# Attention, router and experts on one core: zero fill by GpSimd, a shorter index chain, and four batches written out

## The chip, the cores and the metric

The kernel runs on one core of a Trainium2 chip. The metric is the device time of one execution in microseconds. The core has five engines with a queue of instructions each: TensorE (PE, matmuls and transposes), VectorE (DVE), ScalarE (ACT), GpSimd (POOL) and SyncE (SP). Each runs its queue in order; between engines, order is made by semaphores. Data moves between memory (DRAM) and on-chip SBUF by DMA, issued from the queues of SP, POOL and ACT, and carried by 16 DMA engines. Matmul results land in PSUM, eight banks of 512 float32 for each of 128 partitions.

## The reference

```
scores = scale * q @ k.T;  heads 0-3: local mask, heads 4-7: strided mask   # q,k,v [4, 8, 576, 64]
x = softmax(scores) @ v                                        # as rows [2304, 512]
do = x @ w_skip > 0;  e = argmax(x[do] @ w_gate);  gate = softmax(...)[e]   # 8 experts
x[do] += gate * (relu(x[do] @ w1[e]) @ w2[e])                   # w1 [8,512,1024]
g = leaky_relu(x @ w_in, 0.01);  out = g @ w_out                # w_in [512, 2048]
```

## The kernel before

**Attention.** One batch element is 11 groups of work (`GROUPS`): six local ones (96 queries, g = 0 to 5) and five strided ones (126 rows, the last 72, g = 6 to 10), each for four heads. A group goes PE `scores` (L1322 to L1336) -> DVE `scores_less_max` (L1007, L1014) -> ACT `exps` (L804) -> PE `probs` (a transpose, L1348) -> ACT `probs_out` (L813) -> PE `values` (L1361) -> DVE `normalised` (L1023, L1027, L1034, which writes `xo`). The steps of three neighbouring groups are interleaved. Before a group's scores, q and k of its heads must stand transposed in `qt` and `kt`. That is done in 16 chunks for each batch (`CH`): PE transposes a chunk (L1314), ACT or, for those in `ON_DVE`, DVE copies it out of PSUM (L797, L1000); a chunk of k takes two copies, one of q a single one. `CH_AT` says before which group's scores a chunk is done: chunks 0 to 7 of the next batch at groups 7 to 10, chunks 8 to 11 in `head(b)`, the bridge between two batches, and 12 to 15 at groups 2 to 5. The program has the first batch's head, then a loop of three rounds `rest(b); head(b)`, then the last `rest`.

**Loads and stores of the attention.** SP issues them all, in the order of `batch(b, ...)`, L449: after `xo` of group g is written, the store of `xo` to `x_rows` (at g = 2 and 5 one store for three local groups, at each strided group one), the load of v of the next batch for g (one DMA for a local group, four for a strided one, L401), and at g = 2, 4, 6, 8 the loads of q or k of the batch after next (`q_st`, `k_st`). SP runs a loop for the first two batches, and written-out code for the last two. POOL (and ACT, for half of q) copies `q_st` and `k_st` to `q_in` and `k_in`. `xo` has six slots, so DVE's L1034 waits until the store of the group that used the slot before has landed (L1030 to L1033): group 6 waits for the store of groups 0 to 2 of its own batch, group 9 for that of 3 to 5.

**Router and index chain.** `x_rows` is read back (`x_sb`, L441 to L446), transposed, split in two and multiplied with the gate weights for 18 tiles of 128 rows. Then DVE works out, in steps that each wait for the one before (`step`), which expert takes each row, the rank of the row there, and its place in a list of 160-row tiles, eight tiles with fixed places and up to 14 for overflow. Two one-hot tensors (`oh_tok`, `oh_row`) and 18 matmuls (L1470) turn the places into `tok_idx`, the list of rows by half tile. POOL gathers the rows of tile 0 with it (`gather_x`, `s_plan` at 1).

**Experts and MLP.** Each 160-row tile takes 64 matmuls (L1497, L1513) with weights that SP loads a tile ahead, while POOL gathers the next tile's rows, writes the records of `sort_rows`, and loads and splits the weights of the MLP (`stage_load`, `stage_split`). The MLP runs on all 18 tiles of rows with every product in three parts. `y_rows` from row 1120 on must be zero where no expert writes: SP issues one fill of 4800 KB (L481) behind the loads of the last expert weights.

## Time and profile before

| | |
|---|---|
| median of 3 runs | 772.04 us (771.41 to 774.05) |
| profiled execution | 777.4 us, of which the span of the core is 775.2 us |
| attention, first scores to last `xo` | 22.66 to 156.5 us |
| router | 156.5 to 178.9 us |
| index chain and first gather | 178.9 to 202.0 us |
| experts | 202 to 361 us |
| MLP | 361 to 775.2 us |

All times are from the start of the span. A row of a timeline gives start, duration, engine, line, operation, what it writes and reads, how often, and in brackets the idle time ahead with what ended it. SPq is SP's queue: its durations are those of issuing a DMA, not of the transfer.

### The profile page before, as it was taken

The page shows a single profiled execution, that of the slowest core. Times are in us where ns is not written, and L with a number is a line of the kernel's source. Part 1 is how long each engine was busy: PE and PEld are TensorE (multiplying, and loading weights), DVE is VectorE, ACT ScalarE, POOL GpSimd, SP SyncE. Part 2 cuts the span into 40 slices and gives each one's busy share as a digit, 9 for nine tenths or more (in the row PEclk, how much of TensorE's full clock was granted, in tenths as well). Part 3 has the DMA queues.
Part 4 walks back from the last instruction along what each step waited for, and adds up shares of the span by engine and source line. Part 5 has one row for each costly group of instructions (what it writes and reads, how often), then busy time and mean ns, then how long its engine had stood idle before and what let it go on. Part 6 is the DMA issues. An engine that isn't in the chain of part 4 may idle for free.

```text
span 775.2 us, 12846 instructions
## 1 busy us (share of the span) xinstructions
PE 716.9 (92%) x4628; PEld 664.1 (86%) x4628; DVE 276.2 (36%) x578; ACT 262.0 (34%) x522; POOL 180.5 (23%) x182
## 2 busy tenths in 40 slices
PE   2989979993699999998999999999999999999997
PEld 2878868873699999997999999998989899999986
DVE  4667656757100000003332333233333333332222
ACT  4687666651111112212222223322232322222222
POOL 2120100011686666562100310040031004001000
PEclk9999998986699999999999999999999999999999
DMA  8483746779799999972100210030012004001001
GB/s 175 107 188 100 168 102 171 218 236 229 168 317 341 300 314 338 315 248 64 43 1 0 70 54 1 7 116 1 1 59 63 0 0 122 0 0 41 1 0 41
DMA packets 73112, 91.46 MB, mean 118 GB/s; under 512 B 26704, under 2 KB 47728, under 8 KB 73073
## 3 DMA queue, kind: packets, MB, share of 16 engines
q1 hardware_dynamic: 63969, 66.14, 29.7%
q0 software_dynamic: 8048, 24.79, 11.3%
q8 instruction: 24, 0.39, 0.2%
q10 hardware_dynamic: 1056, 0.02, 0.1%
q14 instruction: 15, 0.12, 0.0%
HBM read 73.91 MB, written 17.01 MB: 117 GB/s over the span
## 4 chain that ended last, share of the span: by engine, by line
PE 74%; SPq 10%; DMA 5%; DVE 3%; issue 3%; ACT 2%; another core or an unknown queue 2%; ACTq 0%; DVEq 0%; POOLq 0%
PE psum L1584 26%; PE psum L1603 26%; PE psum L1497 8%; PE psum L1513 8%; SPq L401 6%; DMA x_rows<-xo 3%; SPq L396 2%; SPq L386 1%; ACT kt L797 1%; PE psum L1336 1%; PE psum L1523 1%; PE psum L1566 1%; DMA x_sb<-x_rows 1%; SPq L409 1%
## 5 line engine op out<-in xcount | busy, mean ns | idle before, releaser
L1584 PE MATMUL psum<-x2h,wih 128*128 128x384 f32 x384 | 130.6, 340 | 1.9 <-DVE x2l L1256 1.9
L1274 DVE SCALAR_TENSOR_TENSOR g_act<-g_raw 128x384 f32<-128x384 f32 x96 | 53.6, 558 | 219.4 <-ACT g_raw L960 205.9
L1584 PE MATMUL psum<-x2h,wil 128*128 128x384 f32 x384 | 129.5, 337 | 0.0
L1584 PE MATMUL psum<-x2l,wih 128*128 128x384 f32 x384 | 129.0, 336 | 0.0
L960 ACT ACTIVATE g_raw<-psum 128x384 f32<-128x384 f32 x96 | 47.2, 492 | 235.3 <-PE psum L1584 232.0
L1603 PE MATMUL psum<-woh,g_l 128*128 128x512 f32 x288 | 114.0, 396 | 0.0
L1603 PE MATMUL psum<-wol,g_h 128*128 128x512 f32 x288 | 113.7, 395 | 0.0
L1603 PE MATMUL psum<-woh,g_h 128*128 128x512 f32 x288 | 112.1, 389 | 0.7 <-DVE g_l L1278 0.7
L1497 PE MATMUL psum<-xt,wring 128*128 128x160 f32 x512 | 80.9, 305 | 0.6 <-issue 0.6
L759 POOL DMA_INDIRECT out_dram<-o_sb,idxo x15 | 15.9, 1061 | 277.8 <-ACT o_sb L955 274.8
L1513 PE MATMUL psum<-hp,wring 128*128 128x160 f32 x512 | 77.6, 299 | 0.0
L1584 PEld LDWEIGHTS psum<-x2h,wih 128*128 128x128 f32 x384 | 72.2, 188 | 5.7 <-DVE x2l L1256 2.1
L1584 PEld LDWEIGHTS psum<-x2l,wih 128*128 128x128 f32 x384 | 72.1, 188 | 3.5
L1497 PEld LDWEIGHTS psum<-xt,wring 128*128 128x128 f32 x512 | 74.0, 194 | 0.8 <-ACT xt L886 0.8
L1278 DVE TENSOR_TENSOR g_l<-g_act,g_h 128x384 fp32r<-128x384 f32 x96 | 53.6, 558 | 56.9 <-ACT g_h L965 55.7
L1513 PEld LDWEIGHTS psum<-hp,wring 128*128 128x128 f32 x512 | 72.2, 190 | 0.2 <-ACT hp L906 0.2
L1584 PEld LDWEIGHTS psum<-x2h,wil 128*128 128x128 f32 x384 | 72.0, 188 | 0.0
L965 ACT ACTIVATE g_h<-g_act 128x384 fp32r<-128x384 f32 x96 | 50.3, 524 | 60.1 <-DVE g_act L1274 57.6
L1603 PEld LDWEIGHTS psum<-woh,g_l 128*128 128x128 f32 x288 | 54.0, 187 | 11.5
L1603 PEld LDWEIGHTS psum<-woh,g_h 128*128 128x128 f32 x288 | 54.1, 188 | 10.0 <-issue 0.7
L1603 PEld LDWEIGHTS psum<-wol,g_h 128*128 128x128 f32 x288 | 54.0, 187 | 9.1
L906 ACT ACTIVATE hp<-psum 128x160 f32<-128x160 f32 x64 | 19.2, 304 | 100.5 <-PE psum L1497 97.1
(177 smaller groups left out, 899.2 us busy)
## 6 DMA issues: line engine op xcount, KB each, us to landing
wring<-in_moe_w_dram SPq DMA_DIRECT2D x64, 512.0 KB, 8.6
y_rows<-zrow SPq DMA_DIRECT2D x1, 4800.0 KB
q_st<-in_q_dram SPq DMA_DIRECT2D x8, 576.0 KB
k_st<-in_k_dram SPq DMA_DIRECT2D x8, 576.0 KB
x_sb<-x_rows SPq DMA_DIRECT2D x4, 1024.0 KB, 6.4
stage<-in_moe_w_in_dram POOLq DMA_DIRECT2D x4, 1024.0 KB, 9.0
stage<-in_moe_w_out_dram POOLq DMA_DIRECT2D x4, 1024.0 KB, 9.2
vs<-in_v_dram SPq DMA_DIRECT2D x20, 128.0 KB, 7.6
```

Source lines behind the costliest of these rows:

```text
L396: eng.dma_start(vs[lo:P, g, :, 0:DH], src).then_inc(s_v[g], 16)
L401: eng.dma_start(vs[0:G["m"], g, h, 0:DH], src).then_inc(s_v[g], 16)
L759: pool.indirect_dma_start(out=out, out_offset=bass.IndirectOffsetOnAxis(ap=idxo[:, j:j + 1].bitcast(U32), axis=0), in_=o_sb[:, j, :], in_o ...
L906: act.activation(hp[:, f % 4, :], bank[f % 2][:, 0:TILE], ACT.Relu).then_inc(s_hp, 1)
L960: act.activation(g_raw[:, f % 2, :], bank[f % 2][:, 0:MT * P], ACT.Copy).then_inc(s_mr, 1)
L965: act.activation(g_h[:, f % 2, :], g_act[:, f % 2, :], ACT.Copy).then_inc(s_mh, 1)
L1274: dve.scalar_tensor_tensor(out=g_act[:, f % 2, :], in0=g_raw[:, f % 2, :], scalar=LEAK, in1=g_raw[:, f % 2, :], op0=ALU.mult, op1=ALU.max) ...
L1278: dve.tensor_tensor(g_l[:, f % 2, :], g_act[:, f % 2, :], g_h[:, f % 2, :].bitcast(F32), ALU.subtract).then_inc(s_ml, 1)
L1497: last = pe.matmul(bank[f % 2][:, 0:TILE], wring[:, 2 * u_, w_], xt[:, T.par, c, :], start=(c == 0), stop=(c == KD - 1))
L1513: last = pe.matmul(Y[:, c, 0:TILE], wring[:, 2 * u_ + 1, w_], hp[:, f % 4, :], start=(f == 0), stop=(f == FC - 1))
L1584: last = pe.matmul(bank[f % 2][:, 0:MT * P], wt[:, c, f * P:(f + 1) * P], xp[:, T.par, c, :], start=(c == 0 and n == 0), stop=(c == KD - 1 ...
L1603: last = pe.matmul(bank[4 + j][:, :], gt[:, f % 2, j * P:(j + 1) * P], wt[:, f // 4, w_], start=(f == 0 and n == 0), stop=(f == FC2 - 1 an ...
```

## The change

Three things at once. (1) The fill of `y_rows` is cut in three (`zero_rows`, 1600 KB each) and issued by POOL, each behind POOL's copy of a batch's first half of q. (2) In the index chain the list for the eight fixed tiles is made by a shorter chain of its own (`rank`, `hid0`, `row0`, `eq_b`, `tok_b`, `row_b`); the overflow part (`row_o`, `tok_o`), the records and the sort positions come behind the plan, and 18 matmuls for it stand in PE's first expert tile. POOL's part of the one-hot tensors goes to DVE. The two halves of the logits are added by a matmul with `comb`. (3) The attention is written out for all four batches, on SP too, in one even pipeline: no `head`; chunks 8 to 15 stand at groups 1 to 4; POOL does all copies of q and k but the first ones; at the start q and k of the first half come in two pairs of heads, DVE takes every second chunk, and POOL does one memset of `kt`. SP loads q and k of a batch together, at groups 1 and 6.

```diff
-        CH_AT = {2: [12], 3: [13], 4: [14], 5: [15], 7: [0, 1], 8: [2, 3], 9: [4, 5], 10: [6, 7]}
-        ON_DVE = {9, 11}
+        CH_AT = {1: [8, 9], 2: [10, 11], 3: [12, 13], 4: [14, 15]}
+        CH_NEXT = {7: [0, 1], 8: [2, 3], 9: [4, 5], 10: [6, 7]}
+        def on_dve(b, n):
+            return n % 2 == 1 if b == 0 and n < 8 else n in (9, 13)
...
+            qk_load(sp, 0, 0, q, q_st, s_qs[0], PAIRS[0])
+            qk_load(sp, 0, 0, k, k_st, s_ks[0], PAIRS[0])
+            qk_load(sp, 0, 0, q, q_st, s_q2, PAIRS[1])
+            qk_load(sp, 0, 0, k, k_st, s_k2, PAIRS[1])
...
-                    if qk_ahead and g in (2, 6):
-                        sp.wait_ge(s_qi[g // 6], b + 2)
-                        qk_load(sp, b + 2, g // 6, q, q_st, s_qs)
-                    if qk_ahead and g in (4, 8):
-                        sp.wait_ge(s_ki[g // 8], b + 2)
-                        qk_load(sp, b + 2, g // 8, k, k_st, s_ks)
+                    if b + 2 < B and g in (1, 6):
+                        qk_next(b + 2, g // 6)
...
-            sp.dma_start(y_d[(E - 1) * TILE:SKIP, :].rearrange("(p c) n -> p c n", p=FILL),
-                         zrow[:, :].unsqueeze(1).to_broadcast([FILL, ZC, D])).then_inc(s_zd, 16)
...
+                        pool.tensor_copy(to, what).then_inc(s_in, 1)
+                        if b and hs == 0 and dst is q_in:
+                            zero_rows(b - 1)
...
+                if i == 0:
+                    pool.wait_ge(s_tok_o, 1)
                 stage_split(i)
...
+            step(dve.tensor_tensor(posn[:, :, :], RANK[:, 0:NT, :], ohb[:, 0:NT, 1:E + 1], ALU.mult))
+            step(dve.reduce_sum(rank[:, :], posn[:, :, :], AX.X))
+            dve.scalar_tensor_tensor(out=h80[:, :], in0=rank[:, :], scalar=float(HALF), in1=half2[:, :],
+                                     op0=ALU.is_ge, op1=ALU.add).then_inc(s_r, 1)
...
+            dve.tensor_tensor(eq_b[:, :, :], free(hid0[:, :], HB3, 2), free(c_half[:, 0:HB], HB3, 1),
+                              ALU.is_equal).then_inc(s_eqb, 1)
+            dve.tensor_tensor(row_b[:, 0:NR, :], free(row0[:, 0:NR], R3, 2), free(c_row[:, :], R3, 1),
+                              ALU.is_equal).then_inc(s_rowb, 1)
...
+                    if first and f == 5:
+                        for hf in range(2):
+                            pe.wait_ge(s_xf[hf], 2)
+                        pe.wait_ge(s_hot_o, 3)
+                        for t in range(NT):
+                            last = pe.matmul(TIDX_O, row_o[:, t, :],
```

On SP, at the start of the loop over batches. Before, in the loop (96x3x256 is the store of three local groups, 128x4x64 the v load of a local group, 72x4x512 four heads of q or k):

```order
L396 DMA vs<-in_v_dram 96x4x64
L396 DMA vs<-in_v_dram 128x4x64
L386 DMA x_rows<-xo 96x3x256
L396 DMA vs<-in_v_dram 128x4x64
L409 DMA q_st<-in_q_dram 72x4x512
L396 DMA vs<-in_v_dram 128x4x64
```

The change, at the same place (SP's rows 17 to 23):

```order
L427 DMA vs<-in_v_dram 96x4x64
L427 DMA vs<-in_v_dram 128x4x64
L440 DMA q_st<-in_q_dram 72x4x512
L440 DMA k_st<-in_k_dram 72x4x512
L417 DMA x_rows<-xo 96x3x256
L427 DMA vs<-in_v_dram 128x4x64 x3
L417 DMA x_rows<-xo 96x3x256
```

The loads of q and k, one behind the first store and one behind the load at g = 4 before, now both stand ahead of that store.

On PE in the first expert tile of the change (L1501 is the hidden layer, L1517 the output share, L1484 the turn of the next tile's rows, L1553 the new matmuls):

```order
L1484 MATMUL psum<-ident,xg 128x80 x8
L1501 MATMUL psum<-xt,wring 128x160 x4
L1517 MATMUL psum<-hp,wring 128x160 x4
L1501 MATMUL psum<-xt,wring 128x160 x4
L1517 MATMUL psum<-hp,wring 128x160 x4
L1553 MATMUL psum<-tok_o,row_o 80x56 x18
L1501 MATMUL psum<-xt,wring 128x160 x4
```

The overflow list is now made inside the tile, behind its sixth hidden step; before, all matmuls of the list stood ahead of the tile (L1470, 80x88 x18).

## Rows read from the trace of the kernel before

**Rows 1.** The page: TensorE's granted clock in 40 slices of 19.4 us
```profile
PEclk9999998986699999999999999999999999999999
```

**Rows 2.** Stretches: busy of each engine, granted clock, DMA share and rate
```profile
22.66:156.50 133.84, 117.84 (x1134) 111.84 (x1132) 90.39 (x231) 93.49 (x165) 17.02 (x9) 0.95 0.60 152
178.90:202.00 23.10, 4.94 (x47) 4.13 (x46) 15.78 (x55) 2.01 (x4) 6.04 (x6) 0.57 0.88 211
```

**Rows 3.** Timeline of SP's queue, the first store and the q load behind it
```profile
37.26 0.37 SPq L386 DMA_DIRECT2D x_rows<-xo  x1
...
38.46 2.92 SPq L409 DMA_DIRECT2D q_st<-in_q_dram  x1
```

**Rows 4.** DMA issues of the stretch 37.2:37.3, KB and us to landing
```profile
x_rows<-xo SPq DMA_DIRECT2D x1, 288.0 KB, 8.3
```

**Rows 5.** The stretch 34.6 to 54.6 (columns as in rows 2)
```profile
34.60:54.60 20.00, 16.37 (x165) 15.28 (x164) 11.55 (x31) 17.23 (x30) 4.30 (x3) 1.00 0.85 194
```

**Rows 6.** Timeline of DVE: xo of (batch, group) (0, 6), (2, 3), (3, 0), (3, 10)
```profile
49.85 0.42 DVE L1034 TENSOR_TENSOR xo<-psum,den 126x256 f32<-126x256 f32 x1
...
110.55 0.42 DVE L1034 TENSOR_TENSOR xo<-psum,den 96x256 f32<-96x256 f32 x1 [5.18 <-DMA x_rows<-xo]
...
135.99 0.42 DVE L1034 TENSOR_TENSOR xo<-psum,den 96x256 f32<-96x256 f32 x1
...
156.08 0.42 DVE L1034 TENSOR_TENSOR xo<-psum,den 72x256 f32<-72x256 f32 x1
```

**Rows 7.** Timeline of SP's queue, four v loads in the loop, and written out
```profile
105.43 3.71 SPq L401 DMA_DIRECT2D vs<-in_v_dram  x4
...
131.81 3.14 SPq L401 DMA_DIRECT2D vs<-in_v_dram  x4
```

**Rows 8.** Groups of instructions on ACT, 31.5 to 64.5 (one batch)
```profile
L797 ACT ACTIVATE kt<-psum 64x288 f32<-64x288 f32 x14 | 9.4, 670 | 0.3 <-PE psum L1314 0.2
L804 ACT ACTIVATE sc<-sc 96x512 f32<-96x512 f32 (+2 forms) x12 | 7.3, 610 | 5.6 <-DVE sc L1014 5.5
L813 ACT ACTIVATE pt<-psum 128x384 f32<-128x384 f32 (+2 forms) x11 | 5.9, 535 | 0.8 <-PE psum L1348 0.7
...
L842 ACT ACTIVATE q_in<-q_st 72x1024 f32<-72x1024 f32 x2 | 2.1, 1050 | 0.8 <-DMA q_st<-in_q_dram 0.8
```

**Rows 9.** Timeline of the start: two copies on DVE, the third group's scores
```profile
6.33 1.44 DVE L989 COPY q_in<-q_st 72x2048 f32<-72x2048 f32 x1 [2.55 <-DMA q_st<-in_q_dram]
...
13.42 1.16 DVE L989 COPY q_in<-q_st 72x2048 f32<-72x2048 f32 x1
...
26.50 0.42 PE L1327 MATMUL psum<-maskb,identb 96*96 96x512 bf16 x1
```

**Rows 10.** Timeline of the index chain on DVE, PE and POOL
```profile
179.06 0.33 DVE L1097 COPY ls<-psum 128x162 f32<-128x162 f32 x1 [1.83 <-PE psum L1441]
...
183.99 0.28 DVE L1126 TENSOR_TENSOR ovc<-psum,c_over 128x112 f32<-128x112 f32 x1 [0.52 <-PE psum L1460]
...
186.21 0.31 DVE L1141 TENSOR_TENSOR posn<-posn,ohb 128x144 f32<-128x144 f32 x1
...
187.11 0.18 DVE L1146 TENSOR_SCALAR hq<-slot 128x18 f32<-128x18 f32 x1
...
188.44 0.90 DVE L1159 TENSOR_TENSOR oh_row<-row,c_row 128x720 bf16<-128x720 f32 x1
...
192.16 0.85 PE L1470 MATMUL psum<-oh_tok,oh_row 128*80 128x88 bf16 x9 [1.10 <-DVE rec L1163]
...
194.62 1.20 POOL L667 DMA_INDIRECT xg<-x_rows,tok_idx  x1 [2.61 <-issue]
```

**Rows 11.** Timeline of the first expert tile, PE and POOL
```profile
199.99 1.42 PE L1480 MATMUL psum<-ident,xg 80*128 80x80 f32 x8 [6.98 <-DMA xg<-x_rows,tok_idx]
...
202.03 5.38 PE L1497 MATMUL psum<-xt,wring 128*128 128x160 f32 x24 [0.63 <-issue]
...
211.56 4.53 POOL L612 TENSOR_TENSOR wil<-stage,wih 128x2048 fp32r<-128x2048 f32 x1
```

More of the change, by code:

```diff
@@ L436, in x_load @@
+            qk_load(sp, 0, 1, k, k_st, s_ks[1])
+            for g in range(3, NL):
+                v_load(sp, 0, g)
+            qk_next(1, 0)
+            for g in range(NL, NG):
+                v_load(sp, 0, g)
+            qk_next(1, 1)
             def x_load(b):
@@ L447, in x_load @@
                                  ).then_inc(s_x[b], 16)
-            def batch(b, qk_ahead, v_ahead):
+            for b in range(B):
                 for g in range(NG):
@@ L828, in rest @@
-            def rest(b, last):
-                for s_ in range(2, NG):
-                    for n in CH_AT.get(s_, []):
-                        if n >= 8:
-                            chunk(b, n)
-                        elif not last:
-                            chunk(b + 1, n)
-                    probs_out(b, s_ - 2)
-                    exps(b, s_)
-                    if s_ in (6, 8) and not last:
-                        act.wait_ge(s_tq, len(CH) * b + len(CH))
-                        act.wait_ge(s_qs[1], 16 * b + 32)
-                        to, what = heads_in(q_in, q_st, 1)
-                        h2 = slice(s_ // 8 * 2, s_ // 8 * 2 + 2)
-                        part = act.activation(to[:, :, h2, :], what[:, :, h2, :], ACT.Copy)
-                        if s_ == 8:
-                            part.then_inc(s_qi[1], 1)
@@ L850, in _ @@
                 chunk(0, n)
-            act.wait_ge(s_vz, 4)
-            head(0)
-            with act.Fori(0, B - 1) as b:
-                rest(b, False)
-                head(b)
-            rest(B - 1, True)
+            for b in range(B):
+                for g in range(NG):
+                    for n in CH_AT.get(g, []):
+                        if b == 0 and n == 8:
+                            act.wait_ge(s_kz, 1)
+                        chunk(b, n)
+                    for n in CH_NEXT.get(g, []):
+                        if b + 1 < B:
+                            chunk(b + 1, n)
+                    if NG * b + g >= 2:
+                        probs_out(*divmod(NG * b + g - 2, NG))
+                    exps(b, g)
+                    if b == 0 and g == 1:
+                        act.wait_ge(s_wg, 32)
+                        act.activation(wgs[:, :, 0:E + 1], wg[:, :, :], ACT.Copy).then_inc(s_wgh, 1)
             for g in (NG - 2, NG - 1):
@@ L1409, in _ @@
             pe.wait_ge(s_cst, POOL_MASKS)
-            head(0)
-            with pe.Fori(0, B - 1) as b:
-                rest(b, False)
-                head(b)
-            rest(B - 1, True)
+            for b in range(B):
+                for g in range(NG):
+                    for n in CH_AT.get(g, []):
+                        chunk(b, n)
+                    for n in CH_NEXT.get(g, []):
+                        if b + 1 < B:
+                            chunk(b + 1, n)
+                    if g in (0, NL):
+                        copied(b, 15 if g else 7)
+                    scores(b, g)
+                    if NG * b + g >= 2:
+                        probs(*divmod(NG * b + g - 2, NG))
+                    if NG * b + g >= 3:
+                        values(*divmod(NG * b + g - 3, NG))
             probs(B - 1, NG - 2)
```

551 lines of the change are left out of this document (273 added, 278 removed).

## The prediction

> **What bounds the kernel now.** I read the stretches of the stages first. The change touches what lies ahead of 202 us; behind it, experts and MLP follow one another on PE, and what comes earlier there moves everything behind it by as much. In the attention [rows 2] PE is busy 118 of 134 us and ACT 93, with a granted clock of 0.95, so nothing is at its limit on average. The waits say what is: DVE's write of xo for batch 2, group 3 sat 5.18 us until a store had landed [rows 6], and the clock's slices show 0.8 and 0.6 there [rows 1]. The store was late because SP was: in the loop four v loads take SP 3.71 us against 3.14 where the code is written out [rows 7], and a strided group has a store of about 0.9 besides, against 2.0 us for a group on the engines: the last batch, with few chunks left, goes from its first xo at 135.99 to its last at 156.08 [rows 6], ten groups in 20.1 us. Of the engines ACT is the fullest per batch: 14 copies of k at 0.67, 7 of q at about the same, 12 exps at 0.61, 11 copies at 0.535 and 2.1 us of q_in [rows 8], 29 us of the 33 looked at. In the index chain [rows 2] PE has 4.9 of 23 us: DVE's one-by-one steps are the path up to the first gather at 194.62, then the gather itself up to 199.99, then tile 0 at 202.03 [rows 10, 11].
>
> **The start.** The first q copy begins when 576 KB have landed, at 6.33, and PE reaches the third group's scores at 26.50 [rows 9]. With pairs of heads the first data are there after 288 KB, and every second chunk is copied by DVE beside ACT. Worked out in turn (load, copy, two transposes, copy, ...), the first scores come at some 15 us; but the third group now has chunks 10 and 11 ahead of it, whose k lands near 18 behind the same bytes as before and is copied by POOL (1.9 us by its present copies): some 20.8. So the pipeline is 5.7 us earlier.
>
> DVE's copies now run beside POOL's memset of kt. The row beside POOL's memsets is 1.44 us, the one without 1.16 [rows 9]: 0.3 us a copy. The Trainium skill (SBUF — State Buffer, "Who interferes with whom") says that such a copy and a GpSimd instruction shut each other out for the whole instruction; by that a copy could wait out the whole memset, about 2 us as DVE does it now. The row shows 0.3, and I take 0.3, which is inside the rounding of the 5.7.
>
> **Most of it is given back at the first store.** xo of group 6 waits for the store of groups 0 to 2. That store was issued at 37.26 and landed 8.3 us later, at 45.5 [rows 3, 4], 4.3 us ahead of xo (0, 6) at 49.85 [rows 6]. SP gets there no earlier now: its 20 strided v loads of batch 0 are issued ahead of it as before. And both loads of q and k for batch 2 now stand ahead of the store, which stood behind it. They are 1.18 MB, at 194 GB/s in this stretch [rows 5] 6 us: the store lands at 51.4. Without it xo (0, 6) would come at 42 (5.7 earlier, and 2 from ACT's lighter load). So DVE, and two groups later PE, stand for some 9 us, and at this point the change is 1.6 us behind.
>
> **From there to the end of the attention.** ACT per batch: 16 copies of k (10.7), 6 of q (4.0), 11 exps (6.7), 11 copies (5.9): 27.3 us against 29. By slots: groups 1 and 2 together 1 q, 4 k and two groups' 2.3 = 5.7, groups 3 and 4 the same, 7 and 8 with 2 q 6.3, 9 and 10 6.0, and 0, 5, 6 three times 2.05 = 6.2: 29.9, and I add 0.4 for the coupling: 30.3 us a batch. From xo (0, 6) to (3, 6) three of these, 90.9, less 2 for what PE and ACT had done ahead in the stall, less 3.2 for the chunks that the last batch has none of, and 7.0 for the four groups left: 92.7, so 144.1. SP needs some 26 us a batch written out and catches up. Further waits for stores I put at 4.5: about 1 at the second batch's group 1 (its slot's store is behind q and k again), 2.5 at its group 6, 1 at the end as now. The attention ends at 148.6 instead of 156.1: **-7.5**. The router (22.4 us) moves with it.
>
> The loops go away on every engine. PE's rows run over the loop's end without a gap that the views show, so I take nothing. The Trainium skill (Runtime: NRT & Kernel Launch, "Instruction fetch mechanics") says that a taken branch out of the fetched window stalls for a fetch; by that rule three such stalls more would go, without a price there.
>
> **The zero fill.** It runs from 167 to 198, at a DMA share of 0.88 and 211 GB/s [rows 2], so a third, 1.64 MB, is 7.8 us of the engines' time. Nothing waits for it now but the gather beside it (5.4 us from issue to PE's first transpose, [rows 10, 11]); alone I take 0.5 less. Moved into the attention (DMA share 0.60, [rows 2]), the first third falls into the slow strided loads, the second and third beside q and k loads. Nothing if they fit the gaps; at most 7.8 each. I put them within the 4.5 above.
>
> **The index chain.** Before the ranks two steps on the logits and two of the choice go, one small one comes: 4 x 0.34 (0.31 and its wait, [rows 10]) less 0.2 = **-1.2**. Behind the ranks it takes 183.99 to some 193.5 to the list, 9.5. Now: two steps of 144 (0.68), five small ones (0.2 each, overlapped, 0.7), eq_b 0.35, row_b 0.82, tok_b 0.37, row_b 0.82 (half a row of 0.90, its overlap taken off), 9 matmuls 0.85, two small 0.45, handover 0.2: 5.3. **-4.2**. With the gather's 0.5, tile 0 starts **5.9** earlier against the router's end, at 196.1 on the old scale. The steps put behind the plan end at about 200.1 on that scale (some 12 us from 188.1); PE first needs them (s_rec, ahead of the first share) three hidden steps into the tile: 196.1 + 5.4 = 201.5. Hidden, with 1.4 us to spare; without it, that much.
>
> **Tile 0 pays.** 18 more matmuls on PE, at the 0.085 of [rows 10] (0.85 for 9, less its drain) 1.5, and a handover: **+1.7**. POOL's first split waits for the list: it ran 209.55 to 216.1 [rows 11] and would end at some 218.3 on the scale on which PE's need of the next gather is at 226.2; the gather takes 2.4 of issue and 6 to land: 227. **+0.8**.
>
> **The sum.** -7.5 - 5.9 + 1.7 + 0.8 = -10.9 from the profiled execution's 777.4 (span 775.2): 766.5. The runs' median is 772.04; the same difference from it gives **761.1 us**.
>
> **The rivals.** (a) Stores don't bind (chance 0.22): DMA takes the mixed load at more than the 194 GB/s, the store lands by 42. Then no 9 us stall and no 4.5: the attention ends near 138, -18, and the time is 750.5. For it: the chain's stretch, with more than one kind of transfer, has 211 GB/s [rows 2], more than the 194. Against: SP's q load of 38.46 took 2.92 us to issue [rows 3], a full queue. (b) The fill is on the path (0.19): the second and third part each delay the stores by most of their 7.8, 7.5 in all: the attention ends as now, and only the chain's 3.4 is left, 768.6. The Trainium skill (SBUF — State Buffer, "A bandwidth-pool intuition that's wrong (but worth ruling out)") adds that a GpSimd DMA can wait for its descriptors beside VectorE's copies; that would shift a part of the fill later. (c) Slower (0.05): each of the last two parts holds the q and k queue for its whole 7.8, the stores behind fall late in each batch, PE idles, and its clock falls as it did at 113 [rows 1], 3 us each. It decides when waits beyond mine pass 10.9 us: 15.6 of fill and an episode of 3 less the 4.5 give 14.1, 775. (d) Nothing measurable (0.03): the same, stopped between, near 771.
>
> **How the numbers follow.** My own case (0.51) has 756 to 767. The range is to leave out 2 in 10: half of (a) and most of (c) and (d), with (b) inside: 751 to 769. A difference of 0.3%, 2.3 us, is about what a measurement of this kernel can tell. Faster by more 0.93, within 0.03, slower 0.04.
>
> **What would show it.** Scores of the third group near 21; the first store landing near 51 with DVE waiting several us for x_rows<-xo at xo (0, 6); xo (3, 10) near 148; one gap of 5 us or less at (2, 3) gone; POOL's gather 10 us behind the logits; no DMA at 200 GB/s in the chain; 18 matmuls of some 1.5 us in tile 0. The prediction is wrong if the store lands by 45 (then (a)), or if xo waits in each batch for stores behind the fill.

## The result, and the profile after

The changed kernel takes **789.94 us** (median of 4 runs, 788.99 to 791.18) against 771.81 us (4 runs, 771.41 to 774.05) of the kernel before: a ratio of 1.023, with a 95% interval of 1.0203 to 1.0256. It is 2.3% slower, where 761.1 us and 1.4% faster were forecast. The profiled execution took 789.15 us, its span 787.1.

The stretches of the changed kernel first: attention up to the router's first transpose, router up to the logits, chain up to tile 0, tiles up to the MLP. Each row has busy us of the engines, granted clock, DMA share and GB/s.

```profile
16.00:172.50 156.50, 123.92 (x1145) 117.68 (x1143) 86.71 (x229) 93.63 (x165) 28.44 (x17) 0.92 0.65 171
172.50:197.60 25.10, 24.97 (x180) 21.56 (x180) 11.97 (x19) 12.45 (x27) 2.62 (x16) 0.88 0.50 164
197.60:213.25 15.65, 4.87 (x46) 4.08 (x47) 13.21 (x51) 1.73 (x4) 3.12 (x4) 0.55 0.17 48
213.25:372.00 158.75, 155.27 (x1182) 154.21 (x1182) 21.81 (x46) 31.88 (x92) 100.34 (x73) 0.99 0.87 280
```

The attention's last xo comes at 172.06 instead of 156.08 [rows 6]: +16.0 us. The router takes 25.1 instead of 22.5 (156.56 to 179.06), the chain from the logits to tile 0 15.6 instead of 23.0 [rows 2, 10, 11]. From tile 0's first hidden matmul to the end of the span it is 573.8 us, against 573.2. 16.0 + 2.6 - 7.3 + 0.6 is 11.9, the difference of the two spans; the medians differ by 18.1, because the profiled execution of before was a long one of its kind (777.4 against 771.8).

Most of that length lies in the attention. Three later runs (`e4_chain_alone`, `e6_chain_split`, `e10_fill_after_gather`, see below) have the attention of before unchanged, and their last xo comes at 151.90, 151.59 and 151.63, 4.2 to 4.5 us ahead of 156.08. Here the last xo of the change, and that of `e6_chain_split`:

```profile
172.06 0.42 DVE L1049 TENSOR_TENSOR xo<-psum,den 72x256 f32<-72x256 f32 x1
```

```profile
151.59 0.42 DVE L1062 TENSOR_TENSOR xo<-psum,den 72x256 f32<-72x256 f32 x1
```

Against such an execution the attention lost some 20 us and not 16. So the chain did what it promised, and the attention lost more than twice that. The timeline of DVE shows where (xo that waited longest, the time that it waited at the end):

```profile
57.20 0.42 DVE L1049 TENSOR_TENSOR xo<-psum,den 126x256 f32<-126x256 f32 x1 [11.04 <-DMA x_rows<-xo]
...
97.61 0.42 DVE L1049 TENSOR_TENSOR xo<-psum,den 126x256 f32<-126x256 f32 x1 [6.71 <-DMA x_rows<-xo]
...
121.13 0.42 DVE L1049 TENSOR_TENSOR xo<-psum,den 96x256 f32<-96x256 f32 x1 [5.67 <-DMA x_rows<-xo]
```

and the view of waits adds them up, for the changed kernel (16 to 172.5 us), with total, times and longest:

```profile
DVE xo L1049 <- DMA x_rows<-xo: 34.0, 10, 11.0
```

and for the kernel before (16 to 156.5 us):

```profile
DVE xo L1034 <- DMA x_rows<-xo: 8.0, 6, 5.2
```

The xo buffer waits 34 us for its stores, where it waited 8. The stores are late because SP, which issues them, is. Its timeline in the changed kernel:

```profile
17.14 22.64 SPq L432 DMA_DIRECT2D vs<-in_v_dram  x20
...
42.37 0.49 SPq L440 DMA_DIRECT2D q_st<-in_q_dram  x1
42.90 0.54 SPq L440 DMA_DIRECT2D k_st<-in_k_dram  x1
43.48 2.92 SPq L417 DMA_DIRECT2D x_rows<-xo  x1
```

and of the kernel before, the same 20 loads:

```profile
17.15 17.39 SPq L401 DMA_DIRECT2D vs<-in_v_dram  x20
```

Two things are to be read there. The 20 strided loads of v took 22.64 us; those of the kernel before, begun at the same time, took 17.39, and its first store went out at 37.26 [rows 3]. And both loads for batch 2 stand ahead of the store, as the prediction said. The store landed at 57.1, not 51.4. While SP worked through the 20 loads, the first third of the fill was in flight. Pool issued it at 24.5, and from issue to landing the three thirds took, by the view of its tile:

```profile
DMA to landing us min/median/max: 12.3/13.7/16.5
```

where the sum had counted 7.8 us each.

### The profile page after: what moved, and what is told of

It reads as the page before. It is cut to its first block, busy times and chain, and to the rows that moved or that the text cites. A ratio compares the mean times of both kernels' runs of the same rounds, so it can differ in the third digit from the quotient of the medians.

```text
span 787.1 us, 12509 instructions
## 1 busy us (share of the span) xinstructions
PE 725.5 (92%) x4664; PEld 673.9 (86%) x4664; DVE 273.8 (35%) x590; ACT 256.7 (33%) x515; POOL 194.1 (25%) x192
## 4 chain that ended last, share of the span: by engine, by line
PE 80%; SPq 6%; DMA 5%; DVE 4%; ACT 2%; issue 2%; ACTq 0%; DVEq 0%
PE psum L1599 26%; PE psum L1618 25%; PE psum L1517 9%; PE psum L1501 9%; DMA x_rows<-xo 5%; SPq L432 4%; PE psum L1378 2%; PE psum L1399 2%; ACT kt L846 2%; PE psum L1440 1%; PE psum L1457 1%; PE psum L1350 1%; SPq L440 1%; PE psum L1527 1%; PE psum L1581 1%
## 5 line engine op out<-in xcount | busy, mean ns | idle before, releaser
L805 POOL DMA_INDIRECT out_dram<-o_sb,idxo x15 | 15.9, 1062 | 278.8 <-ACT o_sb L982 275.7
L1501 PE MATMUL psum<-xt,wring 128*128 128x160 f32 x512 | 80.5, 304 | 0.7 <-issue 0.6
L1517 PE MATMUL psum<-hp,wring 128*128 128x160 f32 x512 | 77.5, 299 | 0.3 <-DVE pos_i L1224 0.3
L1501 PEld LDWEIGHTS psum<-xt,wring 128*128 128x128 f32 x512 | 73.5, 193 | 1.2 <-issue 1.2
L1517 PEld LDWEIGHTS psum<-hp,wring 128*128 128x128 f32 x512 | 72.1, 190 | 0.5 <-issue 0.5
L1399 PE MATMUL psum<-vs,pt 128*96 128x65 f32 (+2 forms) x352 | 42.1, 267 | 16.8 <-DVE xo L1049 14.7
```

Of the source, the lines that this page charges most:

```text
L805: pool.indirect_dma_start(out=out, out_offset=bass.IndirectOffsetOnAxis(ap=idxo[:, j:j + 1].bitcast(U32), axis=0), in_=o_sb[:, j, :], in_o ...
L1399: last = pe.matmul(OP[n % 2][0:G["m"], h, :], pt[0:G["w"], n % 2, h, 0:G["m"]], vs[0:G["w"], g, h, :], start=True, stop=True)
L1501: last = pe.matmul(bank[f % 2][:, 0:TILE], wring[:, 2 * u_, w_], xt[:, T.par, c, :], start=(c == 0), stop=(c == KD - 1))
L1517: last = pe.matmul(Y[:, c, 0:TILE], wring[:, 2 * u_ + 1, w_], hp[:, f % 4, :], start=(f == 0), stop=(f == FC - 1))
```

## The experiments

Three theories. **F**: the fill in the attention slows SP's queue, and with it loads and stores. **O**: the order of the loads does it, q and k ahead of the store. **P**: the pipeline written out evenly is itself slower than the loop. All ratios are to the kernel before, run beside each on the same chip; its median there was 771.8 us beside the change and 772.3 to 773.7 beside the others. Times within a stage come from one profiled execution of each kernel, and three of them (`e1_fill_back`, `e2_order_back`, `e15_back_spread`) have their first xo 1.5 us or more later than the other profiles of the new attention, for a reason told under "The start" below; so differences of a stage of some 2 us between runs mean little.

One thing changed beside what the runs are named for. The fill of before and of `e4_chain_alone`, `e6_chain_split`, `e10_fill_after_gather` and `e11_fill_last` writes 20 rows from each of 120 partitions (`ZC = 20`); to be divisible by three it is 24 rows from each of 100 in the change and in all the others. Both move some 180 to 230 GB/s, but the DMA share from 180 to 184 us is 0.92 in before and 0.63 in `e3_both_back`.

### Fill and order, put back one by one

`e1_fill_back` leaves the changed kernel as it is, but the fill is SP's again, in one piece behind the last weights:

```diff
+            sp.dma_start(y_d[(E - 1) * TILE:SKIP, :].rearrange("(p c) n -> p c n", p=FILL),
+                         zrow[:, :].unsqueeze(1).to_broadcast([FILL, ZC, D])).then_inc(s_zf, 16)
-                        if b and hs == 0 and dst is q_in:
-                            zero_rows(b - 1)
```

> The changed kernel (789.9 us) with the zero fill taken out of the attention: SP issues it in one piece behind the last expert weights, as before. Theory F (the fill keeps the DMA rings full while v, q, k and the stores go by; the first store then lands at 57 instead of 51): the first strided v loads take SP 17.4 us again instead of 22.6, the first store lands near 51.5, the waits of xo for stores fall from 32.6 us in all to about 12, and the time falls by 17 to 21 less 0.5 for the gather beside the fill: 770 to 773. Theory O (the order of q, k and store on SP is the cause, the fill lies in gaps): the waits stay above 25 us and the time at 784 or more.

`e2_order_back` leaves the fill with Pool and puts the loads at their old places:

```diff
-                    if b + 2 < B and g in (1, 6):
-                        qk_next(b + 2, g // 6)
+                    if b + 2 < B and g in (2, 6):
+                        sp.wait_ge(s_qi[g // 6], brought_in(b + 1, g // 6))
+                        qk_load(sp, b + 2, g // 6, q, q_st, s_qs[g // 6])
+                    if b + 2 < B and g in (4, 8):
+                        sp.wait_ge(s_ki[g // 8], brought_in(b + 1, g // 8))
+                        qk_load(sp, b + 2, g // 8, k, k_st, s_ks[g // 8])
```

> The changed kernel with the loads of q and k of the batch after next where they stood before: q behind groups 2 and 6, k behind groups 4 and 8; the fill stays with POOL in the attention. Theory O: the first store lands 6 us earlier (near 51), the wait of 11 us at the first batch's group 6 falls to about 5, those at group 1 of the second and third batch (4.2 and 5.7) go, and so 15 us or more: 772 to 776. Theory F: the stores still stand in full rings behind the fill; 5 us or less are won: 785 or more.

`e3_both_back` has both edits:

> Both of these edits together: attention written out in the even pipeline, short index chain, but fill and order of the loads as before. If fill and order are all that was wrong, the waits for stores fall to about 5 us and the time to 757 to 763, faster than before (771.8). If the even pipeline is itself slower than the old one with its heads (theory P), it stays at 768 or more with few waits of xo.

Measured, with the last xo and the waits of xo for stores from each profile (new order first):

| | median us | ratio (95%) | last xo | waits for stores |
|---|---|---|---|---|
| the change | 789.94 | 1.0230 (1.0203-1.0256) | 172.1 | 34.0 |
| e1: fill back | 779.55 | 1.0077 (1.0050-1.0104) | 156.2 | 11.4 |
| e2: order back | 785.21 | 1.0176 (1.0150-1.0201) | 165.6 | 23.1 |
| e3: both back | 774.73 | 1.0032 (1.0008-1.0056) | 150.3 | 3.8 |

The fill costs 10.4 us with the new order and 10.5 with the old one; the order costs 4.7 with the fill in the attention and 4.8 without it (by the ratios, which take out that the change ran on another chip, 11 to 12 and 3.5 to 4). The two add up, and both F and O are right, F for at least twice as much. The 20 loads of v show F without any store in play. In `e1_fill_back`:

```profile
17.34 17.66 SPq L432 DMA_DIRECT2D vs<-in_v_dram  x20
```

and in `e2_order_back`, where the third is in flight again:

```profile
17.66 21.89 SPq L432 DMA_DIRECT2D vs<-in_v_dram  x20
```

But with both put back the kernel isn't faster than before, though chain and start are in it. So something is left. P has a part of it: the attention ends at 150.3, only 1.3 us ahead of the loop of before. The gather has another: issued at 183.92, it met the fill, and tile 0 started 13.1 us behind it, against 7.4 in the profile of before.

### The chain alone, the fill alone

`e4_chain_alone` is the kernel before with the new index chain and comb (the parts of the change's diff behind the attention), nothing else:

```diff
-                        last = pe.transpose(LOG[:, 2 * j + u, :], lt[:, j % 2, u * P:(u + 1) * P],
-                                            ident[0:LW, 0:LW])
+                        last = pe.matmul(LOG[:, 2 * j + u, :], lt[:, j % 2, u * P:(u + 1) * P],
+                                         comb[:, :], start=True, stop=True)
...
-            step(dve.tensor_copy(ls[:, :, :], LOG[:, :, 0:E + 1]))
-            step(dve.tensor_tensor(ls[:, :, :], LOG[:, :, E + 1:LW], ls[:, :, :], ALU.add))
```

> The kernel before with the index chain of the change alone (comb matmul, short list, overflow list in tile 0); attention and fill as before. The traces put the chain at 15.6 us from logits to tile 0 against 23.0, the router at 25.1 against 22.6 and the MLP the same: 7.3 less 2.5 is 4.8, and the fill beside the gather may give back 0.5: 767.0 to 768.0. If the gather had gained mainly because the fill was gone, 769 or more.

773.44 us (10 runs, 771.62 to 776.21), ratio 1.0008 (0.9992 to 1.0025): no measurable difference. Its gather on Pool, and PE's first transpose of each half and first hidden matmul:

```profile
187.33 1.22 POOL L685 DMA_INDIRECT xg<-x_rows,tok_idx  x1 [31.32 <-issue]
...
194.62 0.79 PE L1525 MATMUL psum<-ident,xg 80*128 80x80 f32 x4 [8.83 <-DMA xg<-x_rows,tok_idx]
...
197.77 0.80 PE L1525 MATMUL psum<-ident,xg 80*128 80x80 f32 x4 [2.35 <-DMA xg<-x_rows,tok_idx]
...
199.14 1.14 PE L1542 MATMUL psum<-xt,wring 128*128 128x160 f32 x3 [0.57 <-issue]
```

The gather goes out 10.0 us behind the logits (177.35), where it was 15.6 [rows 10]. But tile 0 starts 11.8 us behind it, where it was 7.4 [rows 10, 11]. In the changed kernel that is 5.8 (207.49 to 213.25). The gain of the chain (5.6 us) is there, and the gather gives 4.4 of it back, as long as the fill, behind the weights, is still running. The comb matmul, which the edit brings along, costs something too: from the last xo to the logits it is 25.5 us here and 23.0 in before.

`e5_fill_alone` is the kernel before with only the fill moved to Pool's loop:

```diff
-            sp.dma_start(y_d[(E - 1) * TILE:SKIP, :].rearrange("(p c) n -> p c n", p=FILL),
-                         zrow[:, :].unsqueeze(1).to_broadcast([FILL, ZC, D])).then_inc(s_zd, 16)
...
                     pool.tensor_copy(to, what).then_inc(s_in, 1)
+                    if hs == 0 and dst is q_in:
+                        zero_rows(b)
```

> The kernel before with one part alone: the zero fill in three parts from the Pool queue during the attention. Theory D (the transfers of a third slow the SP queue's loads by 4.5 to 5 us in each of three batches, whatever loop order stands around them): the attention ends some 15 us later, the first gather has the DMA engines to itself and gives 2 us back, 784 to 788 us, and the 20 strided v loads of batch 0 take 21 to 23 us instead of 17.4. Rival L (only the new loop is so sensitive; the old one has room between its q and k loads): 772 to 778 us.

790.08 us (4 runs, 788.87 to 792.67), ratio 1.0224 (1.0188 to 1.0261). That is as much as the whole loss of the change and a little more than theory D expected; rival L falls. The loop of before isn't hardier than the new one: its last xo comes at 170.72, some 19 us later than in the three profiles without this fill. Its SP:

```profile
17.14 22.70 SPq L402 DMA_DIRECT2D vs<-in_v_dram  x20
```

`e12_fill_half` asks whether it is the bytes or the issues: half the rows in three parts from Pool, half from SP at the end. Its diff against `e5_fill_alone`:

```diff
-                c0 = b * (ZC // (B - 1))
+                c0 = b * (ZC // (2 * (B - 1)))
+            sp.dma_start(part[:, ZC // 2:ZC, :], zrow[:, :].unsqueeze(1).to_broadcast(
+                [FILL, ZC // 2, D])).then_inc(s_zd, 16)
```

> The kernel before with the fill divided: half of its rows in three parts of half the size from Pool in the attention, the other half from SP behind the weights. The whole of it in the attention gave 790.1 us. Theory D, proportional (bytes cost what they take from the DMA engines): half of 17 to 19 us, 779 to 783 us. Rival T (the loop has slack, and only what goes beyond it costs): under 776 us. Rival Q (each issue costs, by whatever size, the queue of Pool or an interruption): 786 us or more.

779.83 us (4 runs), ratio 1.0103 (1.0071 to 1.0135): +7.5 us for half the bytes, +17 for all. That is proportional within the intervals, as D says; T and Q, as they were put, fall. Some slack isn't excluded: the attention ends at 158.1, 6.5 us later than without a fill in it, for half the bytes, and 19 for all, and the 20 loads took 18.68 us, where they took 16.3 to 17.9 in the runs without and 22.7 with a whole third. The half parts landed after 7.2 to 8.8 us.

### Where else the fill could go

`e6_chain_split` (the chain alone, the fill in two halves on two queues):

```diff
+        def zero_half(eng, u):
+            c0 = u * (ZC // 2)
+            part = y_d[(E - 1) * TILE:SKIP, :].rearrange("(p c) n -> p c n", p=FILL)
+            eng.dma_start(part[:, c0:c0 + ZC // 2, :], zrow[:, :].unsqueeze(1).to_broadcast(
+                [FILL, ZC // 2, D])).then_inc(s_zd, 16)
...
+            zero_half(sp, 0)
...
+            zero_half(act, 1)
             act.wait_ge(s_sh, 1)
```

> The short chain alone in the kernel before, as in the run where it was worth nothing (773.4 us), but the zero fill goes out in two halves, one behind the weights on SP's queue and one on ScalarE's queue after the last router copy. Theory G (the shorter chain is worth nothing because its gather meets the fill, which moves only some 210 GB/s on one queue and ends at 195 to 199 us): the fill is through by about 190 us, the first gather's tile is turned 3.4 to 5 us after its issue instead of 7.3, and the time falls to 767 to 770 us. Rival W (the fill is limited by what it writes, not by its queue): it still ends at 195 us or later, and the time stays at 772 to 774 us.

772.04 us (10 runs), ratio 0.9982 (0.9962 to 1.0002). Mostly rival W: packets of the fill were seen up to some 191 us (193 in `e4_chain_alone`), and the gather issued at 185.11 was turned from 192.48 on, 7.4 us later, as in `e4_chain_alone`. The two queues together moved little more than one does; the first stretch is of `e6_chain_split`:

```profile
176.00:190.00 14.00, 3.28 (x38) 2.93 (x38) 11.68 (x48) 0.67 (x2) 3.04 (x3) 0.54 0.92 230
```

and this one of the kernel before:

```profile
176.00:198.00 22.00, 6.10 (x59) 4.70 (x57) 16.52 (x57) 2.77 (x7) 5.86 (x5) 0.64 0.90 210
```

`e10_fill_after_gather` (loop of before, short chain without comb) holds the fill until the gather has landed:

```diff
+            for hf in range(2):
+                sp.wait_ge(s_gx[hf], 16)
+            sp.dma_start(y_d[(E - 1) * TILE:SKIP, :].rearrange("(p c) n -> p c n", p=FILL),
+                         zrow[:, :].unsqueeze(1).to_broadcast([FILL, ZC, D])).then_inc(s_zd, 16)
             tile(0, 0)
+            sp.wait_ge(s_zd, 32)
```

> The loop of the kernel before, the short chain with the logits turned and added (no comb), and the whole zero fill issued by SP only once both halves of the first gather have landed, waited for after tile 0. Theory G (the chain's gain is taken by the fill that the gather meets): the first gather's tile is turned 3 to 4 us after its issue and the first hidden matmul of tile 0 comes 16 us after the logits instead of 20 to 22. Theory D (the DMA engines were 0.98 busy in the tile stretch, so a fill there delays weights): the stretch of the tiles takes 3 to 12 us longer than 149 us. Together 768 to 778 us; under 768 would speak against D there, and a first gather that still takes 7 us or more against G.

780.12 us (4 runs), ratio 1.0105 (1.0074 to 1.0137), and it shows both sides. The gather, as G says:

```profile
183.71 1.21 POOL L684 DMA_INDIRECT xg<-x_rows,tok_idx  x1 [27.96 <-issue]
```

```profile
186.91 0.79 PE L1525 MATMUL psum<-ident,xg 80*128 80x80 f32 x4 [4.75 <-DMA xg<-x_rows,tok_idx]
...
189.58 2.74 PE L1542 MATMUL psum<-xt,wring 128*128 128x160 f32 x9 [0.57 <-issue]
```

3.2 us to the first transpose, 5.9 to tile 0. And the tiles, from the first to the last hidden matmul, as D says:

```profile
189.58:351.40 161.82, 154.56 (x1138) 153.65 (x1138) 16.97 (x38) 28.96 (x85) 100.76 (x74) 0.95 0.98 302
```

In the kernel before this stretch is

```profile
202.03:351.73 149.70, 149.00 (x1119) 148.47 (x1120) 12.18 (x22) 28.53 (x85) 99.77 (x73) 0.99 0.94 291
```

12.1 us less. PE was idle for 7.3 us of the longer stretch and for 0.7 of the other, and its matmuls took 5.6 us more, at a granted clock of 0.95 against 0.99. All of it is lost ahead of 230 us: SP's queue stood behind the fill, its next four weight loads took from 194.38 to 215.94 to issue, and from 230 us on PE is busy throughout. So this edit shows the price of a fill ahead of weights on SP's queue; a fill on another queue at this place wasn't tried.

`e11_fill_last` issues it all from Pool in the last batch:

```diff
+            pool.wait_ge(s_xo, NG * (B - 1) + 4)
+            pool.dma_start(y_d[(E - 1) * TILE:SKIP, :].rearrange("(p c) n -> p c n", p=FILL),
+                           zrow[:, :].unsqueeze(1).to_broadcast([FILL, ZC, D])).then_inc(s_zf, 16)
             pool.wait_ge(s_xo, NG * B)
```

> The same kernel with the whole zero fill issued by Pool in the fourth batch, after its fourth group (some 140 us), where the v loads are nearly all issued and no later batch waits for a store. Theory D: the fill is through at 165 to 170 us, beside stores, row loads and weights; the last batch and the router lose 1 to 4 us in all, and the gather gives 4 to 6 us back: 767 to 772 us. Rival (the fill does as much harm there as in the first three batches, by the stores of the last groups and the row loads of the router): 776 us or more.

789.74 us (4 runs), ratio 1.0222 (1.0187 to 1.0257). My expectation failed, and the rival is right: the fill took 32.0 us to land, and one xo waited 20 us for a store beside it:

```profile
172.77 0.42 DVE L1057 TENSOR_TENSOR xo<-psum,den 126x256 f32<-126x256 f32 x1 [20.08 <-DMA x_rows<-xo]
```

That the last batch has few loads to issue doesn't help: its xo buffer has as few places as in the others, and a store that lands late stops it.

### The pipeline itself

`e8_pipe_split` is the changed kernel with the old order of loads (as in e2), the fill in two halves at the end (as in e6), and the logits turned and added as before (the diff of e4 the other way round).

> The changed kernel with the q and k loads at their old places, the zero fill in two halves (SP's and ScalarE's queue) at the end of the attention, and the logits turned and added as before instead of multiplied by comb. From the run of both put back (774.7 us): if theory G holds 5 to 6 us less from the gather, and 1 us less from the router (1.8 us of comb's matmuls less 0.7 us of two adds on VectorE), so 767 to 769 us; without G 773 to 774 us. The router then takes 23.7 us from the last xo to the logits, as before, plus nothing.

773.62 us (10 runs), ratio 1.0019 (0.9999 to 1.0039). Stores hardly bind here (1.3 us in all), so this profile shows the pipeline bare, and from one batch's first xo to the next it takes 33.3 us, not the 30.3 of the prediction:

```profile
61.60 0.42 DVE L1057 TENSOR_TENSOR xo<-psum,den 96x256 f32<-96x256 f32 x1
...
94.91 0.42 DVE L1057 TENSOR_TENSOR xo<-psum,den 96x256 f32<-96x256 f32 x1
```

The loop of before takes 31.8 where no store holds it (`e6_chain_split`, second batch, first xo at 65.68 and 97.49). Why is seen on ACT and PE in slot 8, where both chunks of a k pair stand:

```profile
79.25 2.77 ACT L852 ACTIVATE kt<-psum 64x288 f32<-64x288 f32 x4
```

```profile
82.08 0.42 PE L1379 MATMUL psum<-maskb,identb 96*96 96x512 bf16 x1 [1.78 <-ACT kt L852]
```

Four copies in a row, and PE waits for ACT until they are done. In the changed kernel each of slots 2, 4, 8 and 10 has such a pair; the loop of before has them in slots 8 and 10 and once at the batch's start, between other work.

`e9_pipe_slots` puts chunks 8 to 11 into the first slot and 12 to 15 one to a slot, as before (and gives DVE chunks 9 and 11 instead of 9 and 13):

```diff
-        CH_AT = {1: [8, 9], 2: [10, 11], 3: [12, 13], 4: [14, 15]}
+        CH_FIRST = {1: [8, 9], 2: [10, 11], 3: [12, 13], 4: [14, 15]}
+        CH_LATER = {0: [8, 9, 10, 11], 2: [12], 3: [13], 4: [14], 5: [15]}
```

> The same as the pipeline with the two halves of the fill, with one change: from batch 1 on the chunks 8 to 11 of q and k stand in the first slot of the batch and 12 to 15 one to a slot in slots 2 to 5, as in the kernel before, instead of two to a slot in slots 1 to 4. Theory S (two chunks in each of slots 1 to 4 make these slots longer, 33.3 us a batch against 31.9 in the old loop): 1.4 us less in each of three batches, 3 to 5 us less than the other pipeline run. Rival E (the batch is set by the DMA side, loads and stores, wherever the chunks stand): within 1 us of it.

774.41 us (10 runs), ratio 1.0012 (0.9994 to 1.0029), and 34.1 us a batch (97.29 to 131.43): theory S in this form is wrong. Four chunks in one slot of an even pipeline are no better than two in four; the loop of before had probs and values between them.

`e13_pipe_spread` changes only the tables against `e8_pipe_split`, so that no slot has a whole k pair:

```diff
-        CH_AT = {1: [8, 9], 2: [10, 11], 3: [12, 13], 4: [14, 15]}
-        CH_NEXT = {7: [0, 1], 8: [2, 3], 9: [4, 5], 10: [6, 7]}
+        CH_FIRST = {1: [8, 9], 2: [10, 11], 3: [12, 13], 4: [14, 15]}
+        CH_LATER = {0: [8], 1: [9, 10], 2: [11], 3: [12, 13], 4: [14], 5: [15]}
+        CH_NEXT = {6: [0], 7: [1, 2], 8: [3, 4], 9: [5, 6], 10: [7]}
```

> The pipeline run with the fill in two halves at the end (773.6 us, 33.3 us from batch to batch without a wait for a store), with the chunks spread so that no slot has both halves of a k pair: 8, 9+10, 11, 12+13, 14, 15 in slots 0 to 5 from batch 1 on, and 0, 1+2, 3+4, 5+6, 7 in slots 6 to 10. Theory K (two k chunks in one slot are four copies, 2.8 us in a row on ScalarE, and TensorE waits 0.9 to 1.8 us for them three times a batch): 31.5 to 32 us a batch, 768 to 770 us. Rival (the wait only moves to other slots): 33 us a batch and 773 us.

**763.70 us** (4 runs, 761.8 to 768.41), ratio 0.9879 (0.9843 to 0.9915). The one batch without a wait for a store takes 29.8 us (31.5 and 33.2 the other two):

```profile
92.98 0.42 DVE L1061 TENSOR_TENSOR xo<-psum,den 96x256 f32<-96x256 f32 x1
...
122.83 0.42 DVE L1061 TENSOR_TENSOR xo<-psum,den 96x256 f32<-96x256 f32 x1
```

and PE's waits for ACT's copies of q and k fell from 14.0 us in `e8_pipe_split` to 8.8 in the attention. The placement is worth more than I expected of it: 1.4 points of ratio against `e8_pipe_split`, 10 us, and 7.7 us when the kernel ran again (below). PE's shorter waits for copies of k are what theory K said. But the tables also spread the chunks over all 11 slots instead of 8, and no run parts the two. Waits for stores rose in turn from 1.3 to 9.7 us; the next limit is there.

(CH_FIRST is for batch 0, CH_LATER for the others.) The last three runs take this apart: `e14_after_spread` is the change with these tables, `e15_back_spread` is `e3_both_back` with them, `e16_spread_again` is `e13_pipe_spread` once more.

> The changed kernel with one thing different: the chunks of q and k spread over the slots (8, 9+10, 11, 12+13, 14, 15 in slots 0 to 5 from batch 1 on; 0, 1+2, 3+4, 5+6, 7 in slots 6 to 10). Theory K adds to the fill's cost (each of three later batches is 1.5 to 3 us shorter, whatever the DMA side does): 780 to 785 us. Theory D alone (with the fill and the new load order the batch is set by the DMA engines, and a faster loop only waits longer for its stores): 787 us or more.

788.95 us (4 runs), ratio 1.0196 (1.0148 to 1.0243), no measurable difference from the change. K adds nothing there, and D alone is right: the stores are waited for 31.7 us instead of 34.0. A faster loop only waits longer.

> The changed kernel with fill and load order put back and the chunks spread; the fill in one piece, the logits by comb. Without the spread this was 774.7 us. If the placement carries the gain of the spread run: 764 to 767 us. If the two halves of the fill and the plain logits carry a part of it: 768 to 772 us.

769.09 us (7 runs), ratio 0.9929 (0.9901 to 0.9957), against 1.0032 of `e3_both_back`: the placement carries 1 point (5.6 us by the medians, 8 by the ratios).

> The spread run again, for its size: with the fill in two halves and no comb, 763 to 766 us, 1 to 2 us less than the run without these two, since its router is 1.2 to 1.6 us shorter and two adds on VectorE of 0.35 us each come back.

765.91 us (6 runs, 764.01 to 767.14), ratio 0.9888 (0.9854 to 0.9922). The kernel of `e13_pipe_spread` again: **1.1% faster than the kernel before**, and 3.2 us less than `e15_back_spread` on the same chip, more than I put on comb and the halves. Which of the two has the rest wasn't tried; the router's part, by the profiles, is 23.8 us from the first transpose to the reduce with comb (`e15_back_spread`) and 22.1 without. `e15_back_spread` is one of the profiles that started late; whether its other executions did, no row shows.

## Why the prediction was wrong

**The failed step** is "Further waits for stores I put at 4.5", with the fill's price inside it ("Nothing if they fit the gaps; at most 7.8 each. I put them within the 4.5 above"). The waits after the first were 23 us (34.0 less 11.04), and the fill in the attention costs 15 to 19 us of attention, as the ends of e1 against the change (15.9), e3 against e2 (15.3) and e5 against the three profiles with the attention of before (some 19) show. The bound of 7.8 each was taken from a stretch in which the fill ran with little beside it; beside SP's loads a third landed after 12.3 to 16.5 us. A DMA share of 0.6 looked like room for it. It wasn't: in `e12_fill_half` already half the bytes cost 7.5 us. The prediction's own sign of being wrong, "if xo waits in each batch for stores behind the fill", came. Rivals (b) and (c) named the mechanism: (b), given 0.19, had 7.5 us for it and 768.6 in all; (c), given 0.05, took the fill at 15.6, near what was measured, but set it off against 4.5 of other waits, kept all other gains and came to 775 us. (c) reads its fall of the clock "at 113" from rows 1, and the prediction reads "0.8 and 0.6 there"; in slices of 19.4 us the 0.8 is 116 to 136 us, but the two of 0.6 are 174 to 213, router and chain, and say nothing of a wait for a store. (Shorter stretches do show 0.50 from 114 to 120 us.)

**The base.** The 7.5 us that the attention was to gain were taken off a profile whose attention ended 4.5 us late. A part of that were waits that the same code has less of in other executions: xo (2, 3) waited 5.18 us there [rows 6], 3.39, 1.34 and 1.39 in `e4_chain_alone`, `e6_chain_split` and `e10_fill_after_gather`. So what "one gap of 5 us or less at (2, 3) gone" could give was in part not there to be had, and setting the same difference against the median hid it.

**"SP gets there no earlier now"**, so the store lands at 51.4: right that q and k ahead of it cost 6 us (xo (0, 6) comes at 57.20 with the new order and at 51.21 with the old one in `e2_order_back`; without the fill at 52.62 and 46.81), wrong that SP was as fast as before. It came 6.2 us later (43.48), 5.3 of them in the 20 loads, and the store landed at 57.1. The wait was 11.0 us for 9, and it began at 46.2 and not at 42: where no store holds it, in `e8_pipe_split`, xo (0, 6) comes at 45.50.

**"30.3 us a batch"**: 33.3 for the placement of the change. The sum had ACT's work right (27.3 us a batch) but took ACT as busy throughout the slots that have chunks; the k pairs make PE wait, and ACT then waits for PE. With the chunks spread 29.8 was measured in one batch. In `e3_both_back` the two errors met: no first stall of 9 us, but 3 us more a batch, and it ended at 150.3, near the forecast 148.6. This agreement is chance.

**The order of the loads** I priced once, at the first store. It costs 4.7 us in all, also in later batches (xo (1, 6) waits 6.71).

**The start** was right: third scores at 20.53, forecast some 20.8. But the 0.3 us that a copy beside POOL was to cost was luck. In the changed kernel DVE's four copies from `q_st` and `k_st` took 0.69, 0.69, 0.69 and 0.77 us, because none of them met the memset of `kt` (6.99 to 9.11). In the profile of `e1_fill_back`, where the program's start is the same, the second one did, and took 2.65 us:

```profile
6.53 2.12 POOL L633 MEMSET kt<- 128x2432 f32 x1
```

```profile
6.55 2.65 DVE L1067 COPY k_in<-k_st 72x1024 f32<-72x1024 f32 x1 [1.15 <-DMA k_st<-in_k_dram]
```

It was the same in `e2_order_back` (2.57) and `e15_back_spread` (2.41), whose first xo also come late (30.57 and 30.65, and 30.64 in `e1_fill_back`, against 28.3 to 29.0 in the others). Where the copy came first, the memset was the longer one: 2.55 us in `e3_both_back` and 2.65 in `e9_pipe_slots`. The Trainium skill (SBUF — State Buffer, "Who interferes with whom") states that such a copy can take the ports that VectorE shares with GpSimd, and that whichever issues first has them for the whole instruction while the other is fully blocked. These rows agree. The row of 1.44 us in before agrees too, against how the prediction read it: that copy began at 6.33 inside a memset of POOL that ended at 6.69, and the next, of 80x46 elements, begun at 6.75, took 1.09 us, where it takes 0.13 in the changed kernel. The 0.3 was what was left of a short memset.

**The chain** was right in itself (5.4 forecast; 5.6 from the logits to the gather's issue), but "the gather's 0.5" was mis-sized, and it decides what the chain is worth. With the fill out of the way the gather and its turning take 5.8 us to tile 0, beside it 7.4 in before, 11.8 in `e4_chain_alone` and 13.1 in `e3_both_back`. In `e3_both_back`, `e4_chain_alone` and before, packets of the fill are seen up to 197, 193 and 198 us, though the gather goes out at 183.9, 187.3 and 194.6; a gather issued earlier meets more of it. (Whether the fill from 100 partitions holds a gather longer than that from 120 wasn't tried by itself: to PE's first transpose the gather took 8.0 to 11.2 us beside the first and 5.4 to 7.4 beside the second.) In the changed kernel chain and gather together gave 7.3, forecast 5.9.

**The router** "moves with it (22.4)": missed. comb's matmuls are four instructions of 0.61 us for a pair of tiles

```profile
180.93 0.61 PE L1447 MATMUL psum<-comb,lt 18*128 18x9 f32 x4
```

where before there were two of 0.29 together:

```profile
164.41 0.29 PE L1441 MATMUL psum<-ident,lt 18*128 18x18 f32 x2
```

Over nine pairs that is 2.9 us more of PE, near the 2.6 measured; the two steps that it saves on DVE are 0.7.

**Tile 0 pays**: 0.84 us for the 18 matmuls against 1.7, and no stall at the second gather against 0.8. The step behind the plan was late by 0.31 us. All small.

## What to carry to other kernels

A mean DMA share of 0.6 isn't room for a background transfer where one queue issues loads and stores in order: price the transfer by its bytes (17 us for 4.9 MB here), and read from the issue times of that queue (17.4 against 22.7 us for the same 20 loads) what stands behind it. A transfer that hides behind a serial chain sets a floor for what a shorter chain is worth, if the chain ends in a DMA of its own. And in a pipeline of slots spread the jobs so that no slot gives one engine a long run of them (here four copies, 2.8 us); moving chunks between slots was worth 1% here, once the DMA side left room for it. Before a forecast is taken off one profile, compare it with the median of its kernel: here 5 us of the profile were that execution's own.

## What the runs showed of the hardware

- With the fill in flight the core moved 210 GB/s on one queue and 230 on two (rows above), and two ended it only some 2 us sooner, while 397 GB/s were moved in the stretch 168 to 171 us of `e1_fill_back`, where weights were still coming. In the last batch, beside stores and row loads, the fill's 4.9 MB took 32.0 us to land from Pool's queue; from SP's, behind the weights, it was in flight about as long in before (issued at 167.3, last packets at some 198). Why the fill is slower wasn't tried; the rate was about the same from 120 partitions at a DMA share of 0.92 and from 100 at 0.63, so the share of the engines doesn't tell it.
- A DMA that nobody waits for slows the issuing of others: the 20 loads on SP's queue took 16.3 to 17.9 us to issue without a part of the fill on Pool's queue, 18.7 with a sixth of it and 21.9 to 23.0 with a third.
- A copy of VectorE from SBUF to SBUF and a memset of GpSimd didn't run side by side: the copy that began 0.02 us behind a memset of 2.12 us took 2.65 us instead of 0.69 (above). Copies of VectorE out of PSUM did run beside it (two of `kt`, 1.37 us, begun at 8.24 in the changed kernel, against 1.35 without).
- TensorE's granted clock was 0.92 in the mean over the attention against 0.95 before [rows 2]. PE stood from 52 to 56 us, ahead of the first late store, and from 58 to 62 the clock was at its lower level (1.2 GHz):

```profile
52.00:56.00 4.00, 0.00 (x0) 0.00 (x0) 0.00 (x0) 0.00 (x0) 2.49 (x2) 0.96 0.82 201
58.00:62.00 4.00, 4.00 (x23) 3.86 (x24) 3.39 (x10) 2.09 (x4) 0.43 (x1) 0.50 0.81 235
64.00:68.00 4.00, 2.85 (x32) 2.51 (x31) 3.13 (x9) 3.24 (x6) 0.00 (x0) 1.00 0.49 142
```

  It fell in the same way after the waits that ended at 97 and 121 us. Slices of 19.7 us show only the later of these falls (98 to 138 us), and the first not at all:

```profile
PEclk9999988989599999999999999999999999999999
```
